# Turning x on VectorE from blocks of 32 rows, in a three-layer float32 kernel

## The reference, cut to what matters

```python
# layer 1: decayed linear attention, per head; its output, by token, is x (4, 768, 384)
state = alpha[t, :, None] * state + outer(k[t], v[t]);  out[t] = q[t] @ state
# layer 2: mixing; the change is here
theta = x @ w_theta
zr, zi = x * cos(theta), x * sin(theta)
y = w_tok_r @ zr + w_tok_i @ zi            # over the tokens
u = x + y;  u = u + relu(u @ w_ch)
# layer 3: feed forward
h = relu(u @ w_in);  c = conv over 3 tokens of h;  out = (h * sigmoid(c)) @ w_out
```

## Time and profile before

| | |
|---|---|
| median of 3 runs | 533.54 us (531.12 to 534.22) |
| span of the profiled execution | 530.5 us |
| that execution's own time | not listed apart from its span; the fastest run is 0.6 us above the span |
| TensorE busy | 522.1 us, 98% of the span, at granted clock 1.00 |
| VectorE, ScalarE busy | 441.2 us (83%), 287.4 us (54%) |
| DMA | 37163 packets, 56.93 MB |

### The profile page before, as it was taken

How to read it: one execution, slowest core, us unless ns; L and a number is a source line. 1 busy time by engine, 2 the same in 40 slices (tenths; PEclk the granted TensorE clock), 3 DMA queues, 4 the chain that set the end, 5 groups by cost and what they waited for, 6 DMA issues and landing times.

```text
span 530.5 us, 11806 instructions
## 1 busy us (share of the span) xinstructions
PE 522.1 (98%) x4142; PEld 513.2 (97%) x4142; DVE 441.2 (83%) x801; ACT 287.4 (54%) x607; POOL 72.0 (14%) x65
## 2 busy tenths in 40 slices
PE   8999999999999999999999999999999999999997
PEld 7999988999999999999999999999999999999997
DVE  8999996997886759767786777999888888889874
ACT  4889887765534434444344542555555454545353
POOL 5988893000000000000000000000000000000000
PEclk9999999999999999999999999999999999999999
DMA  8999987476131020211062011202020110201011
GB/s 326 336 308 361 313 302 224 120 236 222 40 104 31 17 70 25 96 30 54 15 205 94 1 45 56 80 2 90 0 89 30 59 56 33 89 0 47 0 46 44
DMA packets 37163, 56.93 MB, mean 107 GB/s; under 512 B 3328, under 2 KB 27392, under 8 KB 37120
## 3 DMA queue, kind: packets, MB, share of 16 engines
q1 hardware_dynamic: 34000, 51.65, 29.3%
q10 hardware_dynamic: 3120, 4.72, 2.5%
HBM read 42.20 MB, written 14.16 MB: 106 GB/s over the span
## 4 chain that ended last, share of the span: by engine, by line
PE 92%; SPq 2%; DVE 2%; DMA 2%; issue 1%; ACT 0%; POOL 0%; DVEq 0%; ACTq 0%
PE y_bank L1475 26%; PE y_bank L1534 19%; PE theta_bank L1521 10%; PE x_bank L1521 10%; PE y_bank L1505 7%; PE theta_bank L1462 7%; PE weighed L1372 4%; PE x_sum L1330 3%; PE x_sum L1345 2%; PE turned L1357 2%; SPq L734 1%; PE x_bank L1450 1%; DMA x_in<-x_scratch 1%; PE turned L1377 1%; PE x_sum L1316 1%
## 5 line engine op out<-in xcount | busy, mean ns | idle before, releaser
L1534 PE MATMUL y_bank<-first_w,z 128*128 128x384 f32 x576 | 109.5, 335 | 0.0
L1534 PEld LDWEIGHTS y_bank<-first_w,z 128*128 128x128 f32 x576 | 101.2, 188 | 0.0
L1475 PE MATMUL y_bank<-first_w,z 128*128 128x384 f32 x432 | 78.0, 337 | 0.1
L1475 PE MATMUL y_bank<-rest_w,z 128*128 128x384 f32 x432 | 76.9, 336 | 0.0
L1475 PEld LDWEIGHTS y_bank<-first_w,z 128*128 128x128 f32 x432 | 74.5, 188 | 0.3 <-issue 0.3
L1475 PEld LDWEIGHTS y_bank<-rest_w,z 128*128 128x128 f32 x432 | 74.7, 188 | 0.0
L1045 ACT ACTIVATE out_rows<-theta_bank 128x386 f32<-128x386 f32 x32 | 15.8, 493 | 50.6 <-PE theta_bank L1521 50.5
L1275 DVE TENSOR_SCALAR x_rows<-out_rows,taps 128x384 f32<-128x384 f32 x64 | 26.8, 419 | 19.5 <-ACT out_rows L1045 19.4
L1462 PE MATMUL theta_bank<-theta_w,x_t 128*128 128x384 f32 x216 | 41.6, 336 | 0.1
L1278 DVE SCALAR_TENSOR_TENSOR x_rows<-out_rows,taps,x_rows 128x384 f32<-128x384 f32 x64 | 39.6, 619 | 2.3
L1282 DVE SCALAR_TENSOR_TENSOR z_full<-out_rows,taps,x_rows 128x384 f32<-128x384 f32 x64 | 39.6, 619 | 2.2
(11 more groups left out here) (126 smaller groups left out, 974.9 us busy)
## 6 DMA issues: line engine op xcount, KB each, us to landing
a_in<-in_a_rows SPq DMA_DIRECT2D x15, 390.0 KB, 5.8
k_in<-in_k_rows SPq DMA_DIRECT2D x15, 384.0 KB, 5.7
q_in<-in_q_rows SPq DMA_DIRECT2D x14, 384.0 KB, 5.3
v_in<-in_v_tokens SPq DMA_DIRECT2D x16, 288.0 KB, 4.8
x_in<-x_scratch SPq DMA_DIRECT2D x24, 192.0 KB, 2.5
y<-x_all SPq DMA_DIRECT2D x7, 576.0 KB, 3.2
u_scratch<-u_sum ACTq DMA_DIRECT2D x6, 576.0 KB, 3.5
u_first<-u_scratch SPq DMA_DIRECT2D x4, 577.5 KB, 4.4
```

What stands on the lines that cost most here:

```text
L1475: ins = pe.matmul(y_bank[2 * d + half][:, 0:HALF], z[s % 2][part][zp][:, d * P:(d + 1) * P], mixing_w(part, wp, s)[:, half_tokens(half)], ...
L1534: ins = pe.matmul(out_bank[half][t][:, 0:MODEL], g[k % 4][gp][:, t * P:(t + 1) * P], out_w[wp][f], start=f == 0 and i == 0, stop=f == FF_T ...
```

## The change

Each tile of x is loaded a second time, by `load_blocks`: four DMAs of 32 tokens each, into `x_blocks`, with 32 channels on 32 partitions and runs of 32 tokens (128 bytes). `flip`, one DVE transpose that turns each 32 by 32 block, makes `x_tokens` of it. `turn` and `hold` are gone. The two operations that find the whole turns (before DVE L1172 and L1174) are now done by ACT (`whole_turns`), at the place of `angle`. The scratch that the framework sets aside for dynamic DMAs is made smaller (1024), which gives room for `x_blocks`.

```diff
@@ pair_step(14), SP
             do.refill_piece(1)
             do.load_first(1)
             do.load_first(2)
+            do.load_blocks(0, 0)
+            do.load_blocks(0, 1)
...
@@ pair_tail
-        do.turn(0, 0)
         do.lower(0, 0)
         do.theta_low()
         do.theta(0, 0)
-        do.turn(0, 1)
         do.scan_state(p)
         do.low(0)
-        do.hold(0, 0)
+        do.flip(0, 0)
         do.high(1)
         do.halve(0, 1)
-        do.hold(0, 1)
         do.angle(0, 0)
...
@@ mix_batch
             tile(do.halve, b, s + 2, last)
-            tile(do.hold, b, s + 2, last)
...
             tile(do.angle, b, s + 1, last)
             tile(do.sines, b, s + 1, last)
-            tile(do.turn, b, s + 2, last)
             tile(do.lower, b, s + 2, last)
+            tile(do.flip, b, s + 1, last)
             if isinstance(b, int) and b == 0:
                 do.fill(s)
...
                 do.load_weight(s)
                 if s in STORED_LATE:
                     do.store_late(s)
+            tile(do.load_blocks, b, s + 2, last)
             if s == 4 and not last:
                 do.spare(b)
...
+    x_blocks = ring("x_blocks", 3, [P, MODEL // BLOCK, BLOCK])
...
-            for t in (x_turned, x_low, x_kept):
+            for t in (x_low, x_kept):
                 t.before(sp, b * T + s, 3)
             load_tile(b, s)
+
+        def load_blocks(b, s):
+
+            x_flipped.before(sp, b * T + s, 3)
+            for t in range(P // BLOCK):
+                sp.dma_start(x_blocks[s % 3][t * BLOCK:(t + 1) * BLOCK, :, :],
+                             x_scratch.rearrange("b (n p) t -> b p n t", p=BLOCK)[b, :, :, s * P + t * BLOCK:s * P + (t + 1) * BLOCK]
+                             ).then_inc(blocks_got[s % 3].sem, 16)
...
-        def hold(b, s):
+        def whole_turns(b, s):
             n = b * T + s
-            x_turned.done(act, n)
-            z_done.before(act, n, 2)
-            act.activation(x_tokens[s % 2][:, :], x_bank[:, 0:MODEL], ACT.Copy).then_inc(x_moved.sem, 1)
+            theta_made.done(act, n)
+            z_done.before(act, n, 1)
+            act.activation(turns[:, :], theta_bank[:, 0:MODEL], ACT.Copy, bias=ROUND, scale=1 / (2 * np.pi)).then_inc(turned_by.sem, 1)
+            turned_by.done(act, n)
+            act.activation(turns[:, :], turns[:, :], ACT.Copy, bias=-ROUND).then_inc(whole.sem, 1)
...
         def angles(b, s):
             n = b * T + s
             theta_made.done(dve, n)
-            z_done.before(dve, n, 1)
-            dve.tensor_scalar(turns[:, :], theta_bank[:, 0:MODEL], 1 / (2 * np.pi), ROUND, ALU.mult, ALU.add).then_inc(turned_by.sem, 1)
-            turned_by.done(dve, n)
-            dve.tensor_scalar(turns[:, :], turns[:, :], ROUND, None, ALU.subtract).then_inc(whole.sem, 1)
             whole.done(dve, n)
...
+        def flip(b, s):
+            n = b * T + s
+            blocks_got[s % 3].done(dve, b * (T // 3) + s // 3)
+            z_done.before(dve, n, 2)
+            dve.transpose(x_tokens[s % 2][:, :], x_blocks[s % 3][:, :, :].rearrange("p n t -> p (n t)")).then_inc(x_flipped.sem, 1)
+
         def product(b, s):
             n = b * T + s
             z_low.before(dve, n, 1)
-            x_moved.done(dve, n)
+            x_flipped.done(dve, n)
...
-        def turn(b, s):
-            n = b * T + s
-            x_got[s % 3].done(pe, b * (T // 3) + s // 3)
-            x_moved.before(pe, n, 1)
...
-            for d in range(MODEL_TILES):
-                ins = pe.transpose(x_bank[:, d * P:(d + 1) * P], x_in[s % 3][:, d, :], ident[:, :])
-            ins.then_inc(x_turned.sem, 1)
...
-    nc = bacc.Bacc("TRN2", target_bir_lowering=False, num_devices=1)
+    nc = bacc.Bacc("TRN2", target_bir_lowering=False, num_devices=1, dynamic_dma_scratch_size=1024)
```

More of the change, by code:

```diff
@@ L24 @@
 HALO = 1
+BLOCK = 32
 WIDE = HALF + 2 * HALO
@@ L223 @@
 PLACES = """refill_piece score scan_after scale_k spread cap by_token inside scan_before scale_q mask mask_late select added
-scan_state high bring keep low theta_high theta_low compare waves refill refill_v judge place divert decide store store_half store_late halve hold turn lower theta angle sines
-product round_z fill load load_first load_weight spare prepare mix sums end send join front gate split back_ff fetch""".split()
+scan_state high bring keep low theta_high theta_low compare waves refill refill_v judge place divert decide store store_half store_late halve flip lower theta angle sines
+product round_z fill load load_first load_blocks load_weight spare prepare mix sums end send join front gate split back_ff fetch""".split()
 Work = namedtuple("Work", PLACES, defaults=[nothing] * len(PLACES))
@@ L601, in layer @@
     x_got = [tally(f"x_got{i}", 16) for i in range(3)]
-    x_turned, theta_made, mixed = tally("x_turned", 1, 3), tally("theta_made", 1, 1), tally("mixed", 2, 2)
-    x_high, x_low, x_moved, x_kept = tally("x_high"), tally("x_low", 1, 3), tally("x_moved", 1, 1), tally("x_kept", 1, 3)
+    blocks_got = [tally(f"blocks_got{i}", 16 * (P // BLOCK)) for i in range(3)]
+    theta_made, mixed = tally("theta_made", 1, 1), tally("mixed", 2, 2)
+    x_high, x_low, x_flipped, x_kept = tally("x_high"), tally("x_low", 1, 3), tally("x_flipped", 1, 3), tally("x_kept", 1, 3)
     turned_by, whole, first, second, bounded = (tally(x, 1, 1) for x in ("turned", "whole", "first", "second", "bounded"))
@@ L836, in _ @@
         program(sp, Work(refill_piece=refill_piece, refill=refill, refill_v=refill_v, decide=decide, store=store, store_half=store_half, store_late=store_late, load_first=load_first,
-                         load=load, load_weight=load_weight, spare=spare, prepare=prepare, end=store_u, back_ff=back_ff))
+                         load_blocks=load_blocks, load=load, load_weight=load_weight, spare=spare, prepare=prepare, end=store_u, back_ff=back_ff))
         stored[0].done(sp, BATCH - 1)
@@ L1073, in _ @@
         act.activation(unused[:, :], state_decay[0][:, 0, ENTERED:], ACT.Copy)
-        for t in (x_moved, sized, sined, cosined, z_high, *u_stored, c_high, h_done, gate_done, g_high, evacuated):
+        for t in (turned_by, whole, sized, sined, cosined, z_high, *u_stored, c_high, h_done, gate_done, g_high, evacuated):
             t.open(act)
@@ L1079, in _ @@
         program(act, Work(by_token=by_token, mask_late=mask_late, keep=keep, spread=spread, cap=cap, high=high, theta_high=theta_high, compare=compare, waves=waves,
-                          halve=halve, hold=hold, sines=sines, round_z=round_z, load_weight=load_weight, spare=spare,
+                          halve=halve, angle=whole_turns, sines=sines, round_z=round_z, load_weight=load_weight, spare=spare,
                           prepare=prepare, sums=sums_of, send=send, fetch=fetch, front=front, gate=gating, split=split, back_ff=back_ff))
@@ L1127, in scan_before @@
             if i == 1:
-                for t in (x_low, turned_by, whole, first, second, bounded, z_done, x_kept, u_done, out_done,
+                for t in (x_low, x_flipped, first, second, bounded, z_done, x_kept, u_done, out_done,
                           c_low, conv1_done, conv2_done, conv3_done, gated_done, z_low, g_low, in_low):
@@ L1307, in _ @@
         program(dve, Work(scan_after=scan_after, scan_before=scan_before, place=place, mask=mask, scan_state=scan_state,
-                          divert=divert, lower=lower, angle=angles, fill=fill, product=product, theta_low=theta_low, low=low, round_z=round_z, load_weight=load_weight, sums=sums_of, end=end, spare=spare,
+                          divert=divert, lower=lower, flip=flip, angle=angles, fill=fill, product=product, theta_low=theta_low, low=low, round_z=round_z, load_weight=load_weight, sums=sums_of, end=end, spare=spare,
                           prepare=prepare, fetch=fetch, front=front, gate=gating, split=split))
@@ L1441, in divert @@
             by_state.if_out_of_range(pe, in_range, by_state.path_tensor)
-        def turn(b, s):
-            n = b * T + s
-            x_got[s % 3].done(pe, b * (T // 3) + s // 3)
-            x_moved.before(pe, n, 1)
-            if isinstance(b, int) and b == 0 and s == 0:
-                before_done.done(pe, LAST_PAIR)
-            for d in range(MODEL_TILES):
-                ins = pe.transpose(x_bank[:, d * P:(d + 1) * P], x_in[s % 3][:, d, :], ident[:, :])
-            ins.then_inc(x_turned.sem, 1)
         def theta(b, s):
@@ L1510, in join @@
         def join():
-            x_moved.done(pe, LAST_TILE)
             first.done(pe, LAST_TILE)
@@ L1536, in back_ff @@
                 ins.then_inc(added_up.sem, 1)
-        for t in (x_turned, theta_made, mixed, multiplied, h_made, added_up):
+        for t in (theta_made, mixed, multiplied, h_made, added_up):
             t.open(pe)
@@ L1545, in _ @@
         pe.wait_ge(dve_const, N_DVE_CONST)
-        program(pe, Work(inside=inside, bring=bring, added=added, judge=judge, score=score, divert=divert, turn=turn, theta=theta,
```

(1 more changed line is left out.)

## The result

In 20 runs each, the changed kernel took 535.0 us (534.05 to 538.17) and the kernel before 532.15 us (531.12 to 534.30). The ratio is 1.0053, 95% interval 1.0043 to 1.0063: slower by half a per cent. The forecast was 535.5, worked out as 1.9 us over the kernel before. Measured are 2.85 us between the medians and 2.8 between the profiled spans, 533.3 against 530.5. Three runs had put the kernel before at 533.54; 20 put it at 532.15. The forecast also put the median 3.0 us above the span, from those three runs; the kernel after has 535.0 above 533.3, which is 1.7. So its span of 532.4 was 0.9 too low and the step to the median 1.3 too large, and that the absolute number comes out only 0.5 off is luck.

What follows compares the result with a forecast made beforehand. TensorE, busy 98%, was taken to bound all but batch 0 of the mixing, bound by SP's queue. 7.2 us late there, less 5.6 won back, plus 0.3, gave +1.9 us, about 535.5, range 531 to 541.

Steps and rivals of the forecast that it cites:

- Step 1: Tail before batch 0's mixing: ACT, with the turns added, is late by 0.56 us, and SP's stores shift with it.
- Step 2: SP's queue, batch 0: four block DMAs for tile (0, 2) cost 1.9 us behind the stores; the last lands at 114.8.
- Step 3: Tile (0, 2): transpose 0.50, low part 0.87, products 1.75; mixing begins at 118.0, TensorE idles 5.9 us and is 4.8 late.
- Step 4: Batch 0: the DVE and ACT chain takes 8.0 us per tile against TensorE's 7.8, so mixing (0, 3) begins at 125.95.
- the rival of the clock: TensorE's clock falls behind the idle time before mixing (0, 2): +1 to +5 us on the forecast, chance 24%.
- Step 5: Tile (0, 4): blocks behind the stores land at 131.7, the chain wants them at 130.8; mixing (0, 4) begins at 134.9.
- Step 6: Mixing (0, 5), with no theta before it: the chain needs 8.0 us, so it begins at 142.9, TensorE 7.2 late.
- What is won back: Behind batch 0, tiles (1, 1) to (3, 5): TensorE saves the transposes of 17 groups at 0.33 us, 5.6 us.
- +0.3 at batch ends: At the batch ends DVE has less room: 0.1 us allowed for each of three.
- The packet of 128 bytes: Block loads: unknown price per small packet, taken as 27 ns, so a tile's 1536 packets take 2.6 us of all 16 engines.
- the dear packets: Rival: at 73 ns a packet, blocks (0, 2) and (0, 4) land 3 to 5 us later, +3 to +6 us; chance 13%.
- The blocks are in time: Rival: the flip of tile (0, 2) finds its data by 108.6 us, 22 groups pay, -6.4 us, 527.1; chance 13%.

Runs made afterwards that it cites:

- kernel 3: The changed kernel with the two operations that find the whole turns put back on DVE: median 535.0 us, ratio 1.0056 to the kernel before.
- kernel 2: The changed kernel with 46 transposes into the unused x_bank keeping TensorE busy before mixing (0, 2): median 534.62 us, ratio 1.0039 to the kernel before.
- kernel 9: The changed kernel with the blocks of tile (0, 2) issued right behind those of the first two tiles: median 533.47 us, ratio 1.0021 to the kernel before.
- 11: As kernel 10, with the flip at the head of DVE's iteration: median 527.73 us, ratio 0.9910 to the kernel before.
- kernel 10: As kernel 9, with the 32 late stores issued by GpSimd: median 529.58 us, ratio 0.9943 to the kernel before.
- kernel 1: The changed kernel with the loads of blocks issued ahead of the late stores in SP's queue: median 537.12 us, ratio 1.0100 to the kernel before.
- 8: The changed kernel, all on SP, reordered: flip early, blocks before stores, one pair's store in the tail, weight loads earlier: median 540.37 us, ratio 1.0158 to the kernel before.
- kernel 5: The changed kernel with the 32 late stores issued by GpSimd in place of SP: median 530.57 us, ratio 0.9972 to the kernel before.

## Why the prediction was right, and where it was not

- **Step 1, the tail, +0.56.** Mixing (0, 0) began 0.40 later (96.14 against 95.74). Relative to theta(0, 0), which started 0.49 earlier (0.30 of it is `turn(0, 0)`, which is gone), it is 0.9, and kernel 3 shows that it is ACT's turns (1.45 us of wait with them, 0.56 without). Right in kind, 0.3 low.
- **Step 2, blocks(0, 2).** Forecast: issued 110.8 to 112.3, landed 114.8. Trace: 110.12 to 111.65, landed 114.0. Right; the issue price of 0.48 was 0.50, the stores went faster.
- **Step 3.** Transpose 0.50 (its pitch, 114.03 to 114.53). Mixing forecast at 118.0, began at 117.27; idle time forecast 5.9, was 4.98. Right.
- **Step 4.** The period of DVE's and ACT's chain was 8.0 us by forecast and is 124.31 - 116.57 = 7.74 between the first low parts of z of tiles (0, 2) and (0, 3) in the kernel after. Slightly high, and just below TensorE's own 7.8, so TensorE and the chain share the pace. Mixing (0, 3) was forecast at 125.95 by the chain and began at 127.92: TensorE, at the fallen clock in mixing (0, 2), set it, which only the rival of the clock had.
- **Step 5** did not show in the kernel after: `flip(0, 4)` found its data at 131.64, and mixing (0, 4) began at 135.72, behind TensorE's own work, where 134.9 was forecast. It was not wrong as a mechanism. Kernel 2, where the clock stays full, has it: 1.71 us of wait at 131.0, mixing (0, 4) at 134.24 (forecast 134.9), kernel 9 too.
- **Step 6.** Mixing (0, 5) forecast at 142.9, was 142.68; 7.2 late by forecast, 6.97 by trace. This agreement is in part two things that stand in for each other: the fallen clock for step 5's wait. Without the fall it was 141.97 (kernel 2), 0.9 below the forecast.
- **What is won back** is the mis-sized term. 17 x 0.33 = 5.6 less "+0.3 at batch ends" is 5.3; measured 4.26. The waits of weight loads for `u_sum` and `u_part` grew from 0.2 to 1.9 us. I had allowed 0.1 for each of three batch ends; it was 0.45 each by what was won back (5.6 - 4.26) and 0.57 by the waits. Kernels 3 and 11 show that the part for `u_sum` hangs on DVE's order there: 1.9 and 0.0 in place of 1.1 before `mix`.
- **The sum.** Forecast 7.2 - 5.3 = 1.9; measured 6.97 - 4.26 = 2.7 at mixing (3, 4), and 2.8 on the span.
- **The packet of 128 bytes**, taken as 27 ns. In a steady tile (177 to 180.5 us) the DMA line of the kernel after reads

```profile
q1 hardware_dynamic: 1290, 0.31, 39.4%
```

  0.394 x 3.5 x 16 = 22.1 us of engine time. Less 384 packets of x_in at 27 ns, 10.4, it leaves 11.7 for 906 packets under 512 bytes: 13 ns each, below the rows at 27 and at 73, so the dear packets did not come. The Trainium skill (DMA: Bandwidth & Descriptors, Specifications) has transfers below 512 bytes lose rate. By the byte the trace agrees, 128 in 13 ns against 512 in 27. But the prediction took from it that a packet's price lies above 27 ns, and that does not follow from a lower rate and is not so. Step 2 shows the blocks landing in 2.35 us, so the small packets did not set the time there.
- **The rivals.** The clock did fall (24% given), but as a rival it was +1 to +5 and it came to 0.8 on the span, since step 5's wait took most of it over. So the rival came true as a mechanism and not as a time. "The blocks are in time" (527.1) is what kernels 10 and 11 made true in kind, by moving the stores and one load: medians 529.58 and 527.73, beside a kernel before at 532.36 there. It promised 6.4 us, and they gained 2.8 and 4.6. In kernel 10 the 1.3 us of the batch ends are missing, and at mixing (0, 5) it is 1.46 late where the rival had it 1.1 early (5 x 0.33 - 0.56).

## What to carry to other kernels

Work that was taken off the engine that sets the end was worth nothing here until the data that replace it were there: look for the first place where the new load stands behind other traffic, in the issuing queue and in the DMA engines, and issue it from a point where its source is ready and its buffer free, before the big transfers. A new order within the full stretch of the in-order queue only moved the delay (kernels 1 and 8); a load issued ahead of that stretch helped (9), another idle queue helped (5), both together more (10), and then an operation placed early on VectorE helped as well, which had cost time while its data were late. When a prediction's late points agree with the trace, check each wait by name: here one that was left out had taken the place of one that was counted.

## What the runs showed of the hardware

- Issuing a DMA of 48 KB cost SyncE 0.50 us in a free stretch. Right behind four weight loads of 384 KB, four of them took 3.69 us (kernel 1) and 5.42 us (kernel 5) in place of 2.0, and landing took 5.6 to 6.5 us (kernel 1) and up to 7.33 (kernel 5) in place of 2.35.
- TensorE's clock: behind 4.98 us without work it was granted 0.50 for 5.8 us of matmuls; behind 2.85 us (kernel 5) a mixing lasted 8.05 in place of 6.50; behind 2.22 us (kernel 9) it was granted 0.50 for 2 us; behind 1.66 (kernel 9) a mixing took 6.48, no loss. In the kernel after, the fall cost 2.75 us at its place and 0.8 of the span.
- VectorE turns 128x384 float32 in blocks of 32 in 572 ns, 0.50 from start to start, close to its copy of that size (546).
